# A fused attention and two-layer MoE kernel: the order of preparatory steps in the last block of the first phase

## The reference

```
state = gamma * state + k_t v_t^T ; y_t = (1/8) * q_t state      # 4 batches, 8 heads, 768 steps, 64 dims
h = x @ w_in  (3072x512 @ 512x2048);  g = h if h >= 1, 0 if h <= -1, else (h+1)^2/4 ;  x2 = g @ w_out
h = x2 @ w2_in (3072x512 @ 512x1024); sm = softmax(h) (sum + 1e-9); solu = h*sm
ln = (solu - mean)/sqrt(var + 1e-6) * g_ln ;  out = ln @ w2_out (1024x512)
```

## Time and profile before

| what | value |
|---|---|
| median of 3 runs (858.33 to 858.91) | 858.83 us |
| the profiled execution's own time | 858.88 us |
| its span, first to last instruction | 857.1 us |
| PE busy | 846.3 us, 99% |
| DVE busy | 565.9 us, 66% |
| ACT busy | 360.4 us, 42% |
| POOL busy | 307.9 us, 36% |
| HBM traffic over the span | 158 GB/s |
| mean granted TensorE clock | 0.998 |

### The profile page before, as it was taken

How to read it: one execution, slowest core, us unless ns; L and a number is a source line. 1 busy time by engine, 2 the same in 40 slices (tenths; PEclk the granted TensorE clock), 3 DMA queues, 4 the chain that set the end, 5 groups by cost and what they waited for, 6 DMA issues and landing times.

```text
span 857.1 us, 14555 instructions
## 1 busy us (share of the span) xinstructions
PE 846.3 (99%) x5518; PEld 725.3 (85%) x5518; DVE 565.9 (66%) x1069; ACT 360.4 (42%) x568; POOL 307.9 (36%) x286
## 2 busy tenths in 40 slices
PE   9999999999999999999999999999899999999998
PEld 7788888888988888888988888897688888888886
DVE  4655577666745575555755485579789988898831
ACT  2444342323322243223422243354665766775642
POOL 2687555535332253225212242636541112221000
PEclk9999999999999999999999999999999999999999
DMA  9924358854443435443434337350065654456351
GB/s 340 386 99 145 127 172 302 268 192 148 151 132 125 149 120 166 146 144 115 148 116 144 100 98 245 102 195 25 30 213 178 174 169 149 147 185 182 113 171 63
DMA packets 79621, 136.50 MB, mean 159 GB/s; under 512 B 8000, under 2 KB 26432, under 8 KB 79552
## 3 DMA queue, kind: packets, MB, share of 16 engines
q1 hardware_dynamic: 78976, 135.05, 48.5%
q10 hardware_dynamic: 576, 0.52, 0.2%
HBM read 101.99 MB, written 33.55 MB: 158 GB/s over the span
## 4 chain that ended last, share of the span: by engine, by line
PE 92%; DVE 3%; POOL 2%; issue 1%; ACT 1%; DMA 0%; SPq 0%; DVEq 0%; ACTq 0%; POOLq 0%
PE acc L673 29%; PE h L574 21%; PE o_ps L1505 15%; PE p L1399 13%; PE h L643 5%; PE att L517 3%; PE att L528 2%; PE att L552 1%; PE att L542 1%; DVE x_lo L943 1%; POOL g_lo L1150 1%; DVE w_out_lo L962 1%; DVE h L1027 1%; DMA q<-in_q 0%; DVE g_raw L1019 0%
## 5 line engine op out<-in xcount | busy, mean ns | idle before, releaser
L673 PE MATMUL acc<-g_hi,w 128*128 128x512 f32 x768 | 259.2, 399 | 1.4 <-POOL g_lo L1150 1.4
L1150 POOL TENSOR_TENSOR g_lo<-g_raw,g_hi 128x512 fp32r<-128x512 f32 x96 | 130.7, 1361 | 301.8 <-ACT g_hi L714 301.6
L1027 DVE TENSOR_TENSOR h<-h 128x256 f32<-128x256 f32 x234 | 98.9, 423 | 131.1 <-PE h L574 94.3
L673 PEld LDWEIGHTS acc<-g_hi,w 128*128 128x128 f32 x768 | 144.2, 188 | 37.4 <-issue 3.4
L811 ACT ACTIVATE g_raw<-g_raw,half_bias 128x512 f32<-128x512 f32 x96 | 69.2, 721 | 227.7 <-DVE g_raw L1014 227.7
L673 PE MATMUL acc<-g_lo,w 128*128 128x512 f32 x384 | 150.3, 391 | 0.0
L574 PE MATMUL h<-x_hi,s 128*128 128x256 f32 x596 | 109.3, 281 | 0.0
L714 ACT ACTIVATE g_hi<-g_raw 128x512 fp32r<-128x512 f32 x96 | 60.7, 632 | 90.1 <-DVE g_raw L1019 90.1
L574 PEld LDWEIGHTS h<-x_hi,s 128*128 128x128 f32 x596 | 94.0, 189 | 2.5
L574 PE MATMUL h<-x_hi,w 128*128 128x256 f32 x468 | 87.0, 282 | 0.1
L574 PE MATMUL h<-x_lo,s 128*128 128x256 f32 x298 | 83.7, 281 | 0.0
(11 more groups left out here) (146 smaller groups left out, 1506.6 us busy)
## 6 DMA issues: line engine op xcount, KB each, us to landing
s<-w_sums SPq DMA_DIRECT2D x156, 256.0 KB, 2.7
z<-zq SPq DMA_DIRECT2D x24, 512.0 KB, 2.8
zt<-z SPq DMA_DIRECT2D x92, 128.0 KB, 3.1
kT<-in_kT SPq DMA_DIRECT2D x24, 256.0 KB, 3.0
q<-in_q SPq DMA_DIRECT2D x24, 256.0 KB, 2.8
v<-in_v SPq DMA_DIRECT2D x24, 256.0 KB, 3.6
w_sums<-s_made SPq DMA_DIRECT2D x6, 1024.0 KB, 5.0
x2T<-y SPq DMA_DIRECT2D x24, 256.0 KB, 3.7
```

The costliest lines, as they stand in the source:

```text
L673: last = mm(acc[m][:, :], ww, gg[:, f % 2, :], start=f == 0 and t == 0, stop=f == FT1 - 1 and t == 2)
L1027: tt(out, of_product(p), other, ALU.add).then_inc(sem["taken1"], 1)
L1150: tt(g[1][:, f % 2, :], gate[:, f % 2, :], g[0][:, f % 2, :].bitcast(F32), ALU.subtract)\
```

## The change

It has five parts.

1. b12 of the last block is split by ACT and DVE behind the gate of f = 0 of that block, instead of at the end of block 4 among the other parts.
2. POOL's four sums of w2_in: one each ahead of and behind the low part of f = 4, and one each ahead of and behind that of f = 6, instead of two behind each.
3. DVE's low parts of w2_in and of its sums: in pairs 4, 5 and 6 one behind join 7 and one at the end of the pair, instead of two at the end.
4. In last_steps the gates of f = 14 and 15 go ahead: ACT's w2_out_high of pieces 4 to 7 move behind copy_part(0) and x2_sum_high(1), and x2_sum_high(0) behind the high part of f = 14; on DVE the low parts of w2_out move behind the last gate, and POOL's first sums of x2 behind the low part of f = 13.
5. DVE's low parts of w2_out pieces 2 to 7 are laid among the steps of the second phase's first pair.

```diff
@@ -796,15 +796,11 @@
                 square(LAST, WHOLE - 1)
                 high(LAST, WHOLE - 1)
                 x2_high(0)
-                x2_sum_high(0)
                 square(LAST, WHOLE)
                 high(LAST, WHOLE)
-                for piece in (4, 5):
-                    w2_out_high(piece)
+                x2_sum_high(0)
                 square(LAST, WHOLE + 1)
                 high(LAST, WHOLE + 1)
-                for piece in (6, 7):
-                    w2_out_high(piece)
 
             def square(blk, f):
                 wait(act, sem["clamped"], blk * FT1 + f + 1)
@@ -854,13 +850,15 @@
                 if q:
                     high(*divmod(blk * FT1 + f - 1, FT1))
                 if more:
-                    for name in X_ORDER[1][3:8 if blk + 1 == LAST else 7]:
+                    for name in X_ORDER[1][3:7]:
                         split_part(blk + 1, name)
                 square(blk, f)
                 high(blk, f)
                 if q + AHEAD < FPAIRS:
                     sums_high(q + AHEAD)
                 if blk == LAST:
+                    if p == 0:
+                        split_part(blk, "b12")
                     prepare(p)
 
             act.wait_ge(sem["half_set"], 1)
@@ -877,7 +875,7 @@
                 for p in pairs(blk):
                     pair(blk, p)
             last_steps()
-            finish["act_x2"] = (x2_high, x2_sum_high)
+            finish["act_prepare"] = (w2_out_high, x2_high, x2_sum_high)
             finish["act_evacuate"] = lambda: evacuate(BLOCKS - 1)
 
         @block.vector
@@ -981,30 +979,27 @@
                 tt(mem[name][1][:], mem[f"{name}_raw"][:], mem[name][0][:].bitcast(F32), ALU.subtract)\
                     .then_inc(sem["x2_lo"], 1)
 
-            def prepare(p):
-
-                for kt in {4: (0, 1), 5: (2, 3)}.get(p, ()):
-                    w2_in_low(kt)
+            def prepare(p, n):
+
+                if p in (4, 5):
+                    w2_in_low(2 * (p - 4) + n)
                 if p == 6:
-                    for i in range(2):
-                        w2_sum_low(i)
+                    w2_sum_low(n)
 
             def last_steps():
                 dve.wait_ge(sem["taken1"], 7 * LAST_Q)
                 clamp(LAST, WHOLE - 1)
                 larger(LAST, WHOLE - 1)
                 w2_sum_low(2)
+                clamp(LAST, WHOLE)
+                x2_low(0, "x2_0")
+                larger(LAST, WHOLE)
+                clamp(LAST, WHOLE + 1)
+                x2_low(1, "x2_sum0")
+                larger(LAST, WHOLE + 1)
                 dve.wait_ge(sem["gains"], 16)
                 for piece in range(2):
                     w2_out_lo(piece)
-                clamp(LAST, WHOLE)
-                x2_low(0, "x2_0")
-                larger(LAST, WHOLE)
-                x2_low(1, "x2_sum0")
-                for piece in range(2, 4):
-                    w2_out_lo(piece)
-                clamp(LAST, WHOLE + 1)
-                larger(LAST, WHOLE + 1)
 
             def clamp(blk, f):
                 n = blk * FT1 + f
@@ -1049,6 +1044,8 @@
                 if blk < LAST:
                     attention(blk + 1, 4 * p)
                     attention(blk + 1, 4 * p + 1)
+                if blk == LAST:
+                    prepare(p, 0)
                 if more:
                     for name in ("b11", "b21", "t3"):
                         split_part(blk + 1, name)
@@ -1070,7 +1067,9 @@
                     for n in range(2):
                         sums_low(q + AHEAD, n)
                 if blk == LAST:
-                    prepare(p)
+                    if p == 0:
+                        split_part(blk, "b12")
+                    prepare(p, 1)
 
             def dense(blk):
                 for f in range(FT1):
@@ -1198,30 +1197,25 @@
                 if blk < LAST:
                     attention(blk + 1, 4 * p + 2)
                     attention(blk + 1, 4 * p + 3)
+                if blk == LAST and p in (2, 3):
+                    sum_of_w2(2 * (p - 2))
                 low(blk, f)
                 if blk == LAST and p in (2, 3):
-                    sums_of_w2(p - 2)
-                if blk == LAST and p == 6:
-                    sums_of_x2(0)
-
-            def sums_of_w2(n):
+                    sum_of_w2(2 * (p - 2) + 1)
+
+            def sum_of_w2(n):
 
                 raw, sums = mem["w2_in_raw"], mem["w2_sum_raw"]
                 left, right = slice(0, 512), slice(512, 1024)
                 if n == 0:
                     for kt in range(KT):
                         pool.wait_ge(sem["w2_in_loaded"][kt], 16)
-                    tt(sums[:, 0, :, :], raw[:, 0:2, right], raw[:, 0:2, left], ALU.subtract)\
-                        .then_inc(sem["w2_summed"], 1)
-                    tt(raw[:, 0:2, right], raw[:, 2:4, right], raw[:, 0:2, right], ALU.subtract)\
-                        .then_inc(sem["w2_summed"], 1)
-                else:
-                    pool.wait_ge(sem["w2_summed"], 2)
-                    tt(sums[:, 1, :, :], raw[:, 2:4, right], sums[:, 0, :, :], ALU.subtract)\
-                        .then_inc(sem["w2_summed"], 1)
-                    pool.wait_ge(sem["w2_summed"], 3)
-                    tt(sums[:, 2, :, :], raw[:, 2:4, left], sums[:, 1, :, :], ALU.subtract)\
-                        .then_inc(sem["w2_summed"], 1)
+                wait(pool, sem["w2_summed"], n)
+                out, one, other = ((sums[:, 0, :, :], raw[:, 0:2, right], raw[:, 0:2, left]),
+                                   (raw[:, 0:2, right], raw[:, 2:4, right], raw[:, 0:2, right]),
+                                   (sums[:, 1, :, :], raw[:, 2:4, right], sums[:, 0, :, :]),
+                                   (sums[:, 2, :, :], raw[:, 2:4, left], sums[:, 1, :, :]))[n]
+                tt(out, one, other, ALU.subtract).then_inc(sem["w2_summed"], 1)
 
             def dense(blk):
                 for f in range(FT1):
@@ -1238,8 +1232,8 @@
             def last_steps():
                 for f in range(WHOLE - 1, FT1):
                     low(LAST, f)
-                    if f == WHOLE:
-                        sums_of_x2(1)
+                    if f <= WHOLE:
+                        sums_of_x2(f - WHOLE + 1)
 
             def sums_of_x2(n):
 
@@ -1583,10 +1577,14 @@
                         act.wait_ge(sem["x2_stored"][m], 16 * BLOCKS)
                 copy(o[:, s % 2, :], op[s % 2][:, :]).then_inc(sem["o_ready"], 1)
 
-            x2_high, x2_sum_high = finish["act_x2"]
+            w2_out_high, x2_high, x2_sum_high = finish["act_prepare"]
             copy_part(0)
+            for piece in (4, 5):
+                w2_out_high(piece)
             x2_high(1)
             x2_sum_high(1)
+            for piece in (6, 7):
+                w2_out_high(piece)
             exponential(0, SECOND)
             exponential(0, FIRST)
             squares(0, SECOND)
@@ -1752,23 +1750,28 @@
                     tt(lo, zt[:, s % 2, :, fs, :].rearrange("p i f c -> p f i c"), hi.bitcast(F32), ALU.subtract)\
                         .then_inc(sem["zT_lo"], 1)
 
-            for piece in range(4, FT2):
-                finish["dve_w2_out"](piece)
+            w2_out_lo = finish["dve_w2_out"]
             join_p2(0)
             join_p6(0)
             join_p7(0)
             join_p4(0)
             join_p5(0)
             join_p3(0)
+            for piece in (2, 3):
+                w2_out_lo(piece)
             soften(0, SECOND)
             soften(0, FIRST)
+            for piece in (4, 5):
+                w2_out_lo(piece)
             variance(0, SECOND)
             bias(0, SECOND)
             variance(0, FIRST)
             bias(0, FIRST)
+            w2_out_lo(6)
             turn_squares(0, SECOND)
             finish["dve_evacuate"]()
             turn_squares(0, FIRST)
+            w2_out_lo(7)
             join_p2(1)
             join_p6(1)
             join_p7(1)
```

## The result

The changed kernel takes 861.38 us (median of 15 runs, 859.75 to 862.13) against 858.90 us (15 runs, 857.77 to 859.79) for the kernel before on the same chip: the ratio is 1.0026, 95% interval 1.0018 to 1.0034. It is slower by 2.5 us, and the interval lies above 1. The profiled execution took 861.81 us, its span 860.0. The forecast was 858.9 and no change; the likeliest case did not come.

What follows compares the result with a forecast made beforehand. TensorE was taken to set the time, its largest wait 4.6 us for a ScalarE copy. The terms -0.5 + 2.0 + 0.2 + 0.8 - 5.9 + 3.4 gave 0.0, thus 858.9 against 858.88 us; range 856.2 to 861.2.

Steps and rivals of the forecast that it cites:

- the likeliest case: Whole kernel: the terms sum to no change, 858.9 us, with its own range 857.3 to 860.4; chance 0.38.
- 1, b12 off the gate: Last gate of block 4: without b12's split ahead of its clamp, the gate comes 0.6 earlier: -0.5 us.
- 2, what waits for b12: Pair 2, last block: w2_in issued later delays a sum, so TensorE stalls at product 7: +2.0 us (0.7 to 3.3).
- 3, one sum behind each gate: Gates f=5 to f=7: 0.7 gained at f=5 is taken back at f=7: +0.2 us (-0.7 to +0.6).
- 4, low parts spread: Pair 6: w2_sum_low(0) delays the low part of f=11, lengthening TensorE's wait: +0.8 us (0 to 0.9).
- 5, last gate first: Change-over between the phases: product 7 starts at 600.3 instead of 603.97, at 2.4 GHz: -5.9 us by itself.
- 6, w2_out's low parts in the softmax chain: Second phase's first pair: low parts 2 to 7 lengthen VectorE's critical chain: +3.4 us (2.6 to 4.2).
- the clock rival: Idle ahead of product 7 of pair 2 or product 4 of pair 1 drops TensorE to 1.2 GHz: 860.7; chance 0.17.
- the one with queue and VectorE chain: Queue at its late end in pair 2 and contended VectorE chain together: +1.2 + 0.8, 860.9 us; chance 0.08.
- The signs named for the new profile: Among them: w2_in issued about 521.4, a 2 us w_sums wait near 531, idle ahead of product 4 of pair 1.
- PEclk 1.00 throughout: Sign that TensorE's granted clock stays full; below 1.00 near 534 or 620 would tell of a slower kernel.
- the 2.5 us for the first w2_out step: Second phase: the first w2_out step more than 2.5 us from 629 would tell that the prediction is wrong.

Runs made afterwards that it cites:

- 2: Kernel before with only the move of b12's split behind the gate of f = 0 on both engines: 862.12 us, ratio 1.0035.
- experiment 3: Changed kernel with SP issuing load_w2_in at the end of pair 1, behind pair 2's sums, instead of at the end of pair 0: 858.37 us, ratio 0.9997.
- experiment 5: Changed kernel with five fp32 matmuls of a zeroed tile put ahead of product 7 of pair 2, filling TensorE's wait: 860.90 us, ratio 1.0020.
- experiment 4: Changed kernel with VectorE's low parts of pairs 4 to 6 again two at the end of the pair: 861.03 us, ratio 1.0023.
- experiment 10: On top of experiment 3, last_steps of all three engines and the places of w2_out's parts as in the kernel before: 858.19 us, ratio 0.9989.
- 6: On top of experiment 3, w2_out's low parts 6 and 7 laid behind split_z(0): 856.37 us, ratio 0.9967.
- 7: On top of 6, w2_out's low parts 4 and 5 also laid behind split_z(0): 856.16 us, ratio 0.9969.
- the version that kept the gain (854.7 us): On top of experiment 3: pairs 4 to 6 by twos, first x2 sums as before, VectorE's last gate reordered, pieces 3 to 7 behind split_z(0): 854.74 us.
- 1: Changed kernel with b12 split at the end of block 4 again, on both engines: 858.07 us, ratio 0.9992.

## Where the prediction held and where it failed, step by step

The forecast of no change did not come. The time lies at the top of the stated range: 861.2 is 1.0028 times the 858.83 of before, and the measured ratio is 1.0026 (in microseconds, 861.38 is 0.2 above the bound). The steps are those of the prediction; shifts are of the changed kernel's trace. The last block starts 0.3 us earlier than before, ahead of anything changed.

**1, b12 off the gate** (-0.5): -0.58, and no wait at down step 15. Right.

**2, what waits for b12** (+2.0): +4.0. This is the first failed step. The mechanism was the one worked out: VectorE's split, 1.36 us at 519.57 beside GpSimd, ended at 520.9; SP issued w2_in at 521.00 against 521.4; the first w2_in landed 3.5 us later and the sum 8.7 behind that, where 7.7 had been taken; and TensorE stood idle for 2.23 us ahead of 533.25, inside 0.7 to 3.3. Experiments 2 and 3 show it alone and remove it alone. The wait itself cost 2.4, and what the term left out was the clock, 1.6 more (experiment 5). The clock was held as a rival, with the price about right (1.8) and a chance of 0.17. The rows had a drop after 4.6 us of idle and none after 0.48; nothing excluded one after 2.2. The rule of the Trainium skill ("TensorE: Matmul & The Clock Gate", Part 1), that the clock is withdrawn after idleness, agrees with the trace in kind.

**3, one sum behind each gate** (+0.2): the row at 551.59 has no wait, 0.6 gained, and at 562.55 0.4 is lost again; net -0.2. The mechanism is right in both halves: VectorE's maximum of f = 7 takes 1.22 us at 558.53 beside a GpSimd sum, w2_in_low(0) stands behind it, and the row at 562.55 waits 0.35. In experiment 4, with w2_in_low(0) moved back, that wait is gone.

**4, low parts spread** (+0.8): +0.7, as a wait of 1.17 us at 584.88, where 0.48 stood. Right as a row of TensorE, and not the worth of the part: experiment 4 shows that undoing it, pairs 4 to 6 together, saves 1.3 us there and 0.2 behind the change-over, and in experiment 10, with the last gate in its old place, the copy is 1.2 us earlier, since the clamp of f = 13 no longer waits for two splits. The term should have been followed to the next meeting of the chains.

**5, last gate first** (-5.9): -5.87, from +3.62 at product 1 to -2.25 at the end of product 3. Right: the copy runs at 602.18, with no idle ahead of product 7 and no halved clock behind it.

**6, w2_out's low parts in the softmax chain** (+3.4, bounds 2.6 to 4.2): +5.3. This is the second failed step. The terms were 2.3 for pieces 2 and 3, 1.3 for 4 and 5, 0 for 6 and 0.6 for 7, with a middle taken since some waits would hide them. VectorE's rows in the two traces split the loss. The softening starts 1.0 us earlier than before (611.73 against 612.72) while product 3 ended 2.25 earlier: 1.3 for pieces 2 and 3. The second bias starts 0.2 earlier (618.30 against 618.50): 0.8 for pieces 4 and 5. The first transpose starts 1.0 later (620.14 against 619.11): 1.2 for piece 6. The next join starts 3.0 later (625.59 against 622.60): 2.0 for piece 7. Experiments 6 and 7 agree: 2.9 for pieces 6 and 7, 0.8 for 4 and 5, and 1.6 left for 2 and 3. So pieces 6 and 7 were sized wrong, 0.6 instead of 3, and the others too high. Piece 6 does not lie in a wait: in the kernel before the transpose at 619.11 stands right behind the bias. And both pieces meet GpSimd work on the second x2 load, so that they take 1.30 and 2.05 us. The collision had been looked for at pieces 2 and 3, where GpSimd's work of before stood in view, and not at pieces 6 and 7, though in the kernel before the sums and low part of the next x2 run in that stretch as well.

**The sum**: -0.3 - 0.6 + 4.0 - 0.2 + 0.7 - 5.9 + 5.3 = +3.0, as the row at 631.97 has it. Terms 1 and 3 to 5 were within 0.4; 2 and 6 were short by 2.0 and 1.9 us, and the earlier start and terms 1, 3 and 4 took 0.9 of that back. The forecast of no change rested on the middles of two ranges in which each omission could only add. Of the slower rivals, what the clock rival (860.7) named came. Of the one with queue and VectorE chain (860.9), the chain came beyond its contended end, and the queue did not come at its late end. They had been priced as alternatives, while nothing kept them apart.

**The clock behind the second wait.** The clock rival named the idle ahead of product 4 of pair 1 as well. There the clock fell, and it cost nothing: experiment 3 kept 1.00 in that stretch and loses the same 5.3 us from the end of product 3 to the first w2_out step, with longer waits for VectorE (0.72 and 1.24) in place of the slow matmuls. VectorE's chain set that end.

The signs named for the new profile came, but for PEclk 1.00 throughout and the 2.5 us for the first w2_out step, which is 3.0 off; both were named as what would tell of a slower kernel.

## What to carry to other kernels

Before moving a small instruction, ask what waits for it on an engine that issues DMAs, and in what order that engine's queue then stands: moving 0.7 us of VectorE work cost TensorE 4 us in pair 2, and one line of order on the queue undid it. Price a predicted stall together with the clock that may fall behind it. Work that is moved off a chain must be followed to where it lands: in the traces, terms 5 and 6 cancelled to the tenth of a microsecond, and in the version that kept the gain (854.7 us) the pieces moved last cost 1.9 us, where the change lost 5.3 to its own.

## What the runs showed of the hardware

An idle of 2.2 us on TensorE was followed by the 1.2 GHz level (0.61 and 0.54 at 533 to 537), which cost 1.6 us; keeping the engine busy over the same wait kept 1.00. From the last block on, the traces of all twelve kernels give this list, with the clock of the 4 us that follow:

| idle of TensorE | times | the clock behind it |
|---|---|---|
| 0.6 to 1.5 us | 23 | 1.00 each time |
| 2.2 to 2.3 us | 3 (the change, 2, 4) | fell each time |
| 2.7 us | 5 (the change, 1, 3, 4, 5) | fell in all but experiment 3 |
| 3.5 and 4.6 us | 3 (10; before, 2) | fell each time |

So the length of the wait alone does not decide. The five waits of 2.7 us are the same one, ahead of product 4 of pair 1, and in experiment 3 it left the clock at 1.00:

```profile
618.39 0.47 PE L1393 MATMUL p<-w_sum_hi,x_hi 128*128 128x512 f32 x1 [2.70 <-issue]
```

```profile
618.00:620.00 2.00, 1.61 (x7) 1.38 (x8) 2.00 (x3) 0.42 (x1) 1.51 (x1) 1.00 0.62 250
```

A VectorE pass of 512 columns with two SBUF inputs took 0.68 to 0.74 us alone, 1.30 beside short GpSimd operations and 2.05 beside one of 2.38 us. The Trainium skill ("SBUF — State Buffer", section "Who interferes with whom") has the pair hold each other off for a whole instruction; the row at 623.62 agrees: it began 0.87 us into GpSimd's operation and ended 0.54 us behind the end of that operation. Nearly the same distance stands in four other collisions of the changed kernel: the split at 519.57 and piece 6 at 618.92 ended 0.55 us behind the GpSimd operation that they met, the maxima at 547.29 and 558.53 ended 0.54 behind. In these five rows a pass that met a GpSimd operation took what was left of it, and 0.55 us.
